# Packed 32-wide merges, a tighter inverse and a reordered attention chain inside a fused DeltaNet, MLP and MoE kernel

## The reference, cut to what matters

```python
for t in range(S):                      # attention, per head
    kt, vt, bt = (k_n[:, :, t], v[:, :, t], beta[:, :, t, None])
    y[:, :, t] = einsum('bhd,bhde->bhe', q[:, :, t], state)
    v_old = einsum('bhde,bhd->bhe', state, kt)
    state = state + bt * einsum('bhd,bhe->bhde', kt, vt - v_old)
h = x @ w_in                            # MLP, x = attention output, 3072 x 384
x = maximum(0.01 * h, h) @ w_out
e_idx = argmax(x @ w_gate + modality_bias[modality_id])        # mixture
out[mask] = gate_w[mask] * (relu(x[mask] @ w1[e]) @ w2[e])
```

## Time and profile before

| | us |
|---|---|
| median of 3 runs | 995.38 (991.6 to 998.8) |
| the profiled execution, its own time | 999.67 |
| its span | 997.9 |
| mean granted TensorE clock | 0.935 of 2.4 GHz |
| PE busy | 895.0 (90%) |
| PEld (weight loads) busy | 791.3 (79%) |
| DVE busy | 553.5 (55%) |
| ACT busy | 350.6 (35%) |
| POOL busy | 87.5 (9%) |
| MLP with attention beside it begins | 113.49 |
| mixture begins (first L556) | 714.10 |

### The profile page before, as it was taken

The page is one execution under the profiler, slowest core; times in us unless marked ns, Lnnn a source line. Parts: engine busy times, 40 slices in busy tenths (PEclk is TensorE's granted clock), DMA queues, the critical chain, the costliest instruction groups (busy, mean ns, idle before and its releaser), DMA issues.

```text
span 997.9 us, 26900 instructions
## 1 busy us (share of the span) xinstructions
PE 895.0 (90%) x10524; PEld 791.3 (79%) x10525; DVE 553.5 (55%) x1577; ACT 350.6 (35%) x608; POOL 87.5 (9%) x100
## 2 busy tenths in 40 slices
PE   3797589998999999999999999999988999999962
PEld 3796578876888788878887888788877889898862
DVE  4944797476834985498539863343652333333341
ACT  3245325443345425542545243323511122222230
POOL 1000000000002000200020001010012121222211
PEclk9756699997999999999999999999999999999996
DMA  9902164313503451445143412227141111111122
GB/s 134 321 2 45 30 132 110 82 47 84 104 27 90 98 103 35 90 92 109 28 90 81 88 35 60 71 45 220 41 157 41 40 47 32 47 32 47 32 80 72
DMA packets 148308, 77.92 MB, mean 78 GB/s; under 512 B 112496, under 2 KB 144240, under 8 KB 147824
## 3 DMA queue, kind: packets, MB, share of 16 engines
q1 hardware_dynamic: 144112, 66.98, 28.2%
q0 software_dynamic: 4096, 9.48, 3.0%
HBM read 59.30 MB, written 13.21 MB: 73 GB/s over the span
## 4 chain that ended last, share of the span: by engine, by line
PE 72%; DVE 13%; ACT 6%; DMA 3%; issue 3%; SPq 1%; DVEq 1%; POOL 0%; ACTq 0%; POOLq 0%
PE bank L500 17%; PE bank L485 15%; PE bank L581 10%; PE bank L556 10%; PE bank L566 2%; PE bank L392 2%; PE bank L370 2%; PE bank L518 2%; PE bank L401 1%; PE bank L411 1%; DVE inv_t L1272 1%; DVE g_raw L1341 1%; DVE inv_tmp L1266 1%; ACT diag L970 1%; PE bank L422 1%
## 5 line engine op out<-in xcount | busy, mean ns | idle before, releaser
L500 PE MATMUL bank<-wo_hi,g_hi 128*128 128x392 f32 x384 | 141.3, 368 | 6.5 <-DVE g_lo L1346 3.4
L500 PE MATMUL bank<-wo_lo,g_hi 128*128 128x392 f32 x384 | 133.7, 348 | 0.0
L500 PE MATMUL bank<-wo_hi,g_lo 128*128 128x392 f32 x384 | 133.5, 348 | 0.0
L485 PE MATMUL bank<-x_hi,wi_hi 128*128 128x512 f32 x288 | 119.6, 415 | 13.6 <-DVE x_lo L1337 10.2
L1341 DVE SCALAR_TENSOR_TENSOR g_raw<-g_raw 128x512 f32<-128x512 f32 x96 | 66.2, 690 | 117.5 <-ACT g_raw L1020 117.5
L1020 ACT ACTIVATE g_raw<-bank 128x512 f32<-128x512 f32 x96 | 57.3, 597 | 186.4 <-PE bank L485 186.1
L485 PE MATMUL bank<-x_hi,wi_lo 128*128 128x512 f32 x288 | 115.1, 399 | 0.0
L485 PE MATMUL bank<-x_lo,wi_hi 128*128 128x512 f32 x288 | 115.0, 399 | 0.0
L1027 ACT ACTIVATE g_hi<-g_raw 128x512 fp32r<-128x512 f32 x96 | 60.7, 632 | 111.9 <-DVE g_raw L1341 111.9
L1346 DVE TENSOR_TENSOR g_lo<-g_raw,g_hi 128x512 fp32r<-128x512 f32 x96 | 66.2, 690 | 41.8 <-ACT g_hi L1027 41.7
L500 PEld LDWEIGHTS bank<-wo_hi,g_hi 128*128 128x128 f32 x384 | 74.0, 193 | 12.9 <-issue 5.2
(11 more groups left out here) (211 smaller groups left out, 1539.9 us busy)
## 6 DMA issues: line engine op xcount, KB each, us to landing
wo_lo<-wo_lo_d SPq DMA_DIRECT2D x80, 196.0 KB, 2.4
w_raw<-in_moe_w SPq DMA_DIRECT2D x6, 1536.0 KB, 8.3
x_rows<-stage SPq DMA_DIRECT2D x6, 770.0 KB, 6.8
kq_in_rows<-in_k SPq DMA_DIRECT2D x6, 768.0 KB
k_raw<-in_k SPq DMA_DIRECT2D x24, 192.0 KB, 4.6
vals<-in_v SPq DMA_DIRECT2D x48, 96.0 KB, 3.0
kq_in_rows<-in_q SPq DMA_DIRECT2D x6, 768.0 KB
x_raw<-y_t SPq DMA_DIRECT2D x36, 96.0 KB, 2.4
```

The source lines that it names most:

```text
L485: mm = pe.matmul(bank[0][:], a[:, m, P * f:P * f + P], x[:, m, :], start=(m == 0 and x is x_hi and a is wi_hi), stop=(m == KT - 1 and a is ...
L500: mm = pe.matmul(acc[i][:, 0:DX], g[f % 2][:, P * i:P * i + P], w, start=(f == 0 and k == 0), stop=(f == FT - 1 and k == 2))
```

## The change

1. `merge_x` and `merge_p` fill both their banks at once: groups of even number go to one bank, groups of odd number to the other and to the other half of the partitions, so four tiles take turns. `copy_x` and `copy_p` read that layout (groups `odd::2`). `merge_p` waits for both banks of X and both its fills, `updates` for both banks of P.
2. `INV_AT`: slot 2 gets step 25, slot 3 steps 26 to 30, slot 4 none. `inverse_out` stays in slot 4.
3. `gram_q(n+1, 1)` stands ahead of `up(n, 1)` in slot 0, not behind it.
4. `outputs(n+1, 0)` and its `copy_y` move from slot 10 to the end of slot 8; the first two `keys_t` move from there to slot 9, the last two from the end of slot 9 into slot 10, ahead of `down`. Their copies move along.
5. `state_sum(n+1, 1, 1)` stands right behind `state_sum(n+1, 1, 0)` in slot 12, ahead of `down`; on DVE both `add_s` stand ahead of `norm`.

```diff
-INV_AT = {13: (0, 5), 14: (5, 9), 15: (9, 13), 0: (13, 17), 1: (17, 21), 2: (21, 25), 3: (25, 30), 4: (30, INV)}
+INV_AT = {13: (0, 5), 14: (5, 9), 15: (9, 13), 0: (13, 17), 1: (17, 21), 2: (21, 26), 3: (26, INV)}
...
-            def merge_x(t, m):
+            def merge_x(t):
                 pe.wait_ge(s.tr_ready, t + 1)
-                b, done = fill(("X", t, m))
+                to = [fill(("X", t, odd)) for odd in range(2)]
                 for j in range(16):
-                    for hh in range(2):
-                        mm = pe.matmul(b[low_p(hh), BLK * j:BLK * j + BLK], inv_s[up_p(hh), 16 * m + j, BLK:CH],
-                                       tr[up_p(hh), 16 * m + j, :], start=True, stop=True)
-                mm.then_inc(done, 1)
+                    for odd in range(2):
+                        for hh in range(2):
+                            mm = pe.matmul(to[odd][0][low_p(hh ^ odd), BLK * j:BLK * j + BLK], inv_s[up_p(hh), 2 * j + odd, BLK:CH],
+                                           tr[up_p(hh), 2 * j + odd, :], start=True, stop=True)
+                        if j == 15:
+                            mm.then_inc(to[odd][1], 1)
...
-                pe.wait_ge(*is_drained(("X", t, m)))
-                b, done = fill(("P", t, m))
+                for odd in range(2):
+                    pe.wait_ge(*is_drained(("X", t, odd)))
+                to = [fill(("P", t, odd)) for odd in range(2)]
...
             def updates(t, c):
                 pe.wait_ge(s.td_ev, 4 * t + 4)
-                pe.wait_ge(*is_drained(("P", t, c)))
+                for odd in range(2):
+                    pe.wait_ge(*is_drained(("P", t, odd)))
...
                 cur, nxt, ff = is_set(n + 1), is_set(n + 2), n >= 0
+                if cur and f == 0:
+                    gram_q(n + 1, 1)
                 if ff and f < FT - 1:
                     up(n, f + 1)
...
                     if f == 10:
-                        outputs(n + 1, 0)
                         if n < 0:
                             outputs(n + 1, 1)
...
                     if f == 12:
                         state_sum(n + 1, 1, 0)
+                        state_sum(n + 1, 1, 1)
...
                 if nxt:
+                    if f == 10:
+                        keys_t(n + 2, 2)
+                        keys_t(n + 2, 3)
...
-                    if f == 12:
-                        state_sum(n + 1, 1, 1)
+                    if f == 8:
+                        outputs(n + 1, 0)
                 if nxt:
-                    if f == 8:
+                    if f == 9:
                         keys_t(n + 2, 0)
                         keys_t(n + 2, 1)
-                    if f == 9:
-                        keys_t(n + 2, 2)
-                        keys_t(n + 2, 3)
...
                     if f == 12:
+                        if cur:
+                            add_s(n + 1, 1, 0)
+                            add_s(n + 1, 1, 1)
                         norm(n + 2)
```

More of the change, by code:

```diff
@@ L312, in eight @@
             return slice(8 * m, 8 * m + 8)
-        def sixteen(m):
-            return slice(16 * m, 16 * m + 16)
         def chunk(c):
@@ L394, in gram_q, with merge_p @@
                 mm.then_inc(done, 1)
-            def merge_x(t, m):
+            def merge_x(t):
                 pe.wait_ge(s.tr_ready, t + 1)
-                b, done = fill(("X", t, m))
+                to = [fill(("X", t, odd)) for odd in range(2)]
                 for j in range(16):
-                    for hh in range(2):
-                        mm = pe.matmul(b[low_p(hh), BLK * j:BLK * j + BLK], inv_s[up_p(hh), 16 * m + j, BLK:CH],
-                                       tr[up_p(hh), 16 * m + j, :], start=True, stop=True)
-                mm.then_inc(done, 1)
-            def merge_p(t, m):
+                    for odd in range(2):
[4 more added lines that the diff above has]
+                            mm.then_inc(to[odd][1], 1)
+            def merge_p(t):
                 pe.wait_ge(s.td_ev, 4 * t + 2)
-                pe.wait_ge(*is_drained(("X", t, m)))
-                b, done = fill(("P", t, m))
+                for odd in range(2):
+                    pe.wait_ge(*is_drained(("X", t, odd)))
+                to = [fill(("P", t, odd)) for odd in range(2)]
                 for j in range(16):
[L410 to L413, removed]
+                    for odd in range(2):
+                        for hh in range(2):
+                            mm = pe.matmul(to[odd][0][up_p(hh ^ odd), BLK * j:BLK * j + BLK], tr[low_p(hh), 2 * j + odd, :],
+                                           inv_s[low_p(hh), 2 * j + odd, BLK:CH], start=True, stop=True)
+                        if j == 15:
+                            mm.then_inc(to[odd][1], 1)
             def old_values(t, c):
@@ L597, in slot @@
                 if cur:
-                    if f < 3:
+                    if f in (1, 2):
                         gram_q(n + 1, f + 1)
                     if f == 5:
-                        merge_x(n + 1, 0)
-                        merge_x(n + 1, 1)
+                        merge_x(n + 1)
                     if f == 6:
-                        merge_p(n + 1, 0)
-                        merge_p(n + 1, 1)
+                        merge_p(n + 1)
                     if f == 7:
@@ L984, in copy_diag, with copy_p @@
                                    ).then_inc(s.td_ev, 1)
-            def copy_p(t, m):
-                act.wait_ge(*is_filled(("P", t, m)))
+            def copy_p(t, odd):
+                act.wait_ge(*is_filled(("P", t, odd)))
                 for hh in range(2):
-                    mm = act.activation(inv_s[up_p(hh), sixteen(m), BLK:CH],
-                                        att_bank(("P", t, m))[up_p(hh), :].rearrange("p (g t) -> p g t", g=16), ACT.Copy)
-                mm.then_inc(drain(("P", t, m)), 1)
+                    mm = act.activation(inv_s[up_p(hh), odd::2, BLK:CH],
+                                        att_bank(("P", t, odd))[up_p(hh ^ odd), :].rearrange("p (g t) -> p g t", g=16), ACT.Copy)
+                mm.then_inc(drain(("P", t, odd)), 1)
             def copy_u(t, c, odd):
@@ L1553, in slot @@
                     if f == 12:
+                        if cur:
+                            add_s(n + 1, 1, 0)
+                            add_s(n + 1, 1, 1)
                         norm(n + 2)
-                if cur and f == 12:
+                if cur and not nxt and f == 12:
                     add_s(n + 1, 1, 0)
```

22 lines of the change are left out of this document (11 added, 11 removed).

## The result

| | us | ratio to the kernel before |
|---|---|---|
| kernel before, 14 runs beside it | 994.67 (991.24 to 1000.68) | |
| changed kernel, 14 runs | 1002.59 (996.75 to 1011.83) | 1.0077, interval 1.0048 to 1.0105 |
| changed, its profiled execution | 1000.28, span 998.5 | |

One run of the changed kernel, 1011.83, was a slow one and is left out of the ratio and its interval.

The account below looks back on a forecast made before the run. PE was taken to bound the kernel (busy 90% of the span, 72% of the chain), DVE next. Terms 5.0 + 0.4 + 0.8 - 1.5 - 1.8 - 2.0 - 1.65 - 0.7 = -1.45 us took 995.38 to about 994.0, range 984 to 1002.

Parts of the forecast that it names:

- Pace of the merges: Four-tile merges stay near 17 ns a record: 0.15 us saved in each of 10 at full clock, -1.5 us.
- the rival built on it (982): Merges halve in time with four tiles, 1.0 us saved each instead of 0.15: 982 us, chance 0.08.
- The longer wait in n = -1: Before the first up, merge_p and updates wait for both banks' copies with no cover: +5.0 us (3.5 to 7).
- `merge_p` behind `sub_w`: In later sets, merge_p's second fill waits for the first sub_w's drain: 0.4 us in one set, +0.4 us.
- Inverse: Slot 4 without step 30 starts the transpose for merge_x 0.45 us earlier in four sets: -1.8 us.
- Clock behind the merges: Shorter idle time ahead of merges avoids two clock falls behind them: -2.0 us (0 to -3.5).
- Boundaries: Parts 3 and 5 at block boundaries: 0.55 us passes at each of three, -1.65; -0.7 at 0 to 1.
- Part 4: gram_k(0) waits 0.2 us for keys copied in the same slot, in four sets: +0.8 us.
- The rival with the clock at the boundary (1006): Clock falls at a new 1.3 us wait ahead of down(n+1, 0) at three boundaries: 1006 us, chance 0.07.

Follow-up runs that it names:

- e10: The changed kernel with old_values(t, 0) and its two sub_w one slot later; 996.41 us, against 1000.69 for the changed kernel beside it.
- e16: The changed kernel with inverse steps 5 to 12 (DVE work in slots 14 and 15) left out; 981.53 us, ratio 0.9865 to the kernel before.
- e3: The changed kernel without part 1, merges as before; 998.15 us, against 1003.77 for the changed kernel beside it.
- e7: The changed kernel without part 1, merges as before, run again in another job; 998.77 us, against 1001.31 for the changed kernel beside it.
- e12: The changed kernel without part 5, second state sum and add_s where they were before; 1000.47 us, against 1000.69 for the changed kernel beside it.
- e8: The changed kernel without part 4, outputs of chunk 0 and key transposes as before; 997.68 us, against 1001.31 for the changed kernel beside it.

## Why the prediction was wrong, term by term

The time missed by 8.6 us, and errors of both signs partly hid each other. In front of the first `up` I had put +5.0 and the traces have +1.5; over the blocks the other terms make -6.45 and the traces have +4.7. The step that failed is the idle time of PE in the blocks. I had -2.95 for it (-1.8 for the inverse, -1.65 and -0.7 at the boundaries, +0.4 for `sub_w`, +0.8 for the keys); it grew by 11.4, which is more than the 9.3 us that the merges saved.

- **Pace of the merges (-1.5): mis-sized, toward less gain.** I read 17 ns a record as the floor of four tiles, because the two-tile merge and the four-tile Gram happened to meet there. The packed merge takes 10 ns a record, 0.93 us less each, -9.3 for ten and 1.7 less in each of the two of n = -1. The two rows were of different shapes: 32x32 against 48x64. (The paces without their tails are also off by a little: 0.2 us less gives 15.7 and 15.0 ns, not 15.9 and 14.9.) The 12 ns a record that I had as an estimate of a floor was undercut too. The Trainium skill ("TensorEngine Tiling (Array Packing)", section Theoretical Speedup) gives the tiling factor as an upper limit of the speedup. The trace agrees: twice the tiles gave 1.73 times the pace at full clock and 1.88 at half, near that limit of two, which I had set aside. But the rival built on it (982) was wrong as well: PE's work fell nearly as it says, and the time didn't follow.
- **The longer wait in n = -1 (+5.0): place right, size wrong.** 3.06 and 2.62 us were forecast as 3.0 and 2.4. From the start of `merge_x` to `updates` it is 9.55 us now and was 7.07: 2.5 later instead of 5.3, since the merges themselves paid back the rest. The first `up` is 1.5 us later on average.
- **`merge_p` behind `sub_w` (+0.4): wrong.** I had PE arrive as `sub_w` begins, and charged one set. PE arrives earlier, because `merge_x` is shorter, and waits 1.2 us in every set, 5.9 in all. e10 is 4.3 us quicker with both moved, though its idle time is about the same.
- **Inverse (-1.8): right.** 0.64 us is left of 1.1, and the total fell from 6.3 to 3.9.
- **Clock behind the merges (-2.0): not there.** With the shorter wait n = 2 still falls behind `merge_p`: `down` at 378.97 takes 0.53 us a matmul. I had read one trace, in which 4 of 5 sets fall; the three others of before have 2, 1 and 1. The four of the changed kernel have 2, 4, 3 and 1.
- **Boundaries (-1.65, -0.7): mechanism right, gain absent.** The wait moved ahead of `down(n+1, 0)` with 1.25 us (1.3 forecast), and e16 shows DVE as its cause. The 0.55 us that I let pass was taken by a wait for g_lo that the sum doesn't have, 0.53 ahead of the last `down` of n = 1, 2 and 3. At n = 0 the same comes as 1.01 and 1.06 us in slots 14 and 15. These come with part 5, not with the merges: e3 and e7 have them, e12 has not.
- **Part 4 (+0.8): too small.** 3.6 us by e8. The wait I costed is there (0.3 to 0.4 us a set); the stops that came with it are not in the sum.
- **No term at all: PE standing still without a wait.** 2.0 us before, 7.5 now. Most of the growth is at two places, 1.4 to 2.5 us in n = 1 that come with part 4 and 1.2 to 2.5 in n = 4 that come with parts 4 and 5. The earlier trace rows has "issue" at 3% of the chain, and I never asked where it lies.
- **The rival with the clock at the boundary (1006)** came near in time by another way: that is luck. Behind the 1.25 us at 343.54 a matmul takes 0.34 us, so no fall there. It falls behind `merge_p` in n = 2 and behind the stop in n = 4.

Shown: which waits went and came; that DVE's work is what PE waits for at the boundaries, and that in n = -1 and n = 0 less of it makes the kernel shorter; that part 5 trades one wait for another of the same size; that the stop in n = 4 needs parts 4 and 5 together. Not shown: how the rest of the 6 to 8 us divides among the parts, since of the runs that leave a part out only e3 and e8 have an interval apart from the changed kernel's, and parts 2 and 3 were never left out by themselves; and what PE lacks in the stops. The stops of the changed kernel differ in length (0.4 to 2.6 us). Those in n = 1 and n = 4 stand at the same record in all four traces, the others come and go at a few fixed records.

## What to carry to other kernels

Before a saving on the busiest engine is put into a sum, ask at each place what ends its next wait: here 9 us of matmul work went, and PE was idle for 11 us more (DVE at the boundaries, `sub_w` behind the merges, stops without a wait). Taking a wait away didn't help by itself either: in e16 the waits at the boundaries went and blocks 1 to 4 kept their length. Look for time in which the busiest engine waits for nothing, find its places in several traces, and read how often the clock falls from several traces too. And trace both kernels several times and time them in several jobs before a difference of 1% is given a sign.

## What was unexpected of the hardware

- Four tiles of 32x32 in turn take fp32 matmuls at 10 ns a record (1.28 us for 128) at full clock and 15 ns at half; two tiles take 17 and 28.
- PE stops for 0.2 to 2.7 us with nothing to wait for, at fixed places of a program. 39 of 44 stops of more than 1 us end 2.2 to 3.6 us after a 16 KB transfer of instructions begins. Behind 1.63, 1.90 and 2.45 us in one place the clock was about 0.55 to 0.6 for the next 3.6 us; behind 1.21 and, in e3, 2.22 us in the same place it stayed at 1.00.
- One program has two levels, 995 and 1008 us, from job to job and on one chip, with a mean clock of 0.940 and 0.935; its neighbours with small edits don't show them (the changed kernel has 1000.7 to 1003.8 in the same jobs).
